# Row-sum guard, accumulator eviction, value products of 384 and 256 columns and the turning of the dense stage's tokens, changed together in a one-core transformer block

## The reference

```
q_rot, k_rot = (rotate(q), rotate(k))
scores = scale * np.matmul(q_rot, k_rot.transpose(0, 1, 3, 2))
attn = np.exp(scores - np.max(scores, axis=-1, keepdims=True))
attn = attn / (np.sum(attn, axis=-1, keepdims=True) + 1e-09)
x = np.matmul(attn, v)                         # then tokens x 512
...
h = np.maximum(x[mask] @ w1[e], 0.0)           # x 8 experts, one per token
y[mask] = gate_w[mask, None] * (h @ w2[e])
...
h = y @ w_in                                   # 512 -> 2048
return (h - np.tanh(h)) @ w_out                # 2048 -> 512
```

## Time and profile before

| | us |
|---|---|
| median of 3 runs | 1150.19 |
| lowest and highest run | 1147.87, 1151.51 |
| the profiled execution | 1149.18 |
| its span, first to last instruction | 1147.4 |
| attention, 0 to 377 | 377 |
| routing, 377 to 450 | 73 |
| experts, 450 to 704 | 254 |
| dense stage, 704 to the end | 443 |

### The profile page before, as it was taken

One profiled execution on the slowest core, in us unless ns is written; L12 is line 12 of the kernel. 1 busy time (PEld: TensorE's weight loads), 2 busy tenths in 40 slices (PEclk: granted clock), 3 DMA queues, 4 the chain that ended last, 5 costly groups with the idle time before them and its releaser, 6 DMA issues. The chain is left out here.

```text
span 1147.4 us, 18602 instructions
## 1 busy us (share of the span) xinstructions
PE 994.0 (87%) x5428; PEld 863.2 (75%) x5429; DVE 622.2 (54%) x1210; ACT 579.8 (51%) x1257; POOL 416.0 (36%) x246
## 2 busy tenths in 40 slices
PE   1988988888899108999999994999999999999996
PEld 1777877778788107888888873887988989889895
DVE  4677777777776433111111112776666666666664
ACT  2666666666665523222222223665556665555553
POOL 3988778768720164706975505000000000000000
PEclk9999999999999558999999997999999999999999
DMA  8776676666532165412542106121000000000001
GB/s 233 197 212 169 182 185 164 185 181 165 146 93 90 25 240 211 156 46 91 161 162 98 56 27 186 55 65 47 1 1 27 0 27 0 0 27 0 28 1 28
DMA packets 63077, 113.82 MB, mean 99 GB/s; under 512 B 20032, under 2 KB 24640, under 8 KB 61120
## 3 DMA queue, kind: packets, MB, share of 16 engines
q1 hardware_dynamic: 52352, 92.62, 27.8%
q10 hardware_dynamic: 7808, 11.31, 3.0%
q0 software_dynamic: 2880, 9.44, 2.4%
HBM read 60.58 MB, written 24.41 MB: 74 GB/s over the span
## 5 line engine op out<-in xcount | busy, mean ns | idle before, releaser
L1413 PE MATMUL hd_ps<-y_hi,w_hi 128*128 128x384 f32 x384 | 131.7, 343 | 4.9 <-DVE g_sb L1579 4.6
L601 DVE TENSOR_REDUCE neg_max<-ps 128x1 f32<-128x576 f32 x144 | 108.2, 751 | 40.3 <-PE ps L371 37.7
L1413 PE MATMUL hd_ps<-y_lo,w_hi 128*128 128x384 f32 x384 | 130.0, 339 | 0.0
L1413 PE MATMUL hd_ps<-y_hi,w_lo 128*128 128x384 f32 x384 | 129.8, 338 | 0.0
L1481 ACT ACTIVATE mag<-hd_ps 128x384 f32<-128x384 f32 x96 | 47.2, 492 | 159.8 <-PE hd_ps L1413 156.9
L1431 PE MATMUL o_ps<-w_hi,g_hi 128*128 128x512 f32 x288 | 114.9, 399 | 6.4 <-DVE g_lo L1588 5.7
L617 DVE TENSOR_TENSOR pt_lo<-ps,pt_hi 128x512 fp32r<-128x512 f32 x144 | 98.5, 685 | 39.9 <-ACT pt_hi L534 39.2
L514 ACT ACTIVATE probs<-ps,neg_max 128x576 f32<-128x576 f32 x128 | 95.4, 745 | 46.6 <-DVE neg_max L601 46.3
L1588 DVE TENSOR_TENSOR g_lo<-g_sb,g_hi 128x384 fp32r<-128x384 f32 x96 | 53.5, 557 | 116.8 <-ACT g_hi L1496 116.8
L534 ACT ACTIVATE pt_hi<-ps 128x512 fp32r<-128x512 f32 x144 | 86.8, 603 | 54.3 <-PE ps L418 54.2
L1431 PE MATMUL o_ps<-w_hi,g_lo 128*128 128x512 f32 x288 | 114.1, 396 | 0.0
(11 more groups left out here) (210 smaller groups left out, 2507.2 us busy)
## 6 DMA issues: line engine op xcount, KB each, us to landing
w_stage<-in_w SPq DMA_DIRECT2D x32, 512.0 KB, 3.8
raw_qk<-in_qk SPq DMA_DIRECT2D x14, 1152.0 KB, 6.1
k_hh<-qk_hi SPq DMA_DIRECT2D x64, 144.0 KB, 2.8
k_ll<-qk_lo SPq DMA_DIRECT2D x64, 144.0 KB, 2.9
sorted_rows<-zeros SPq DMA_DIRECT2D x28, 256.0 KB, 6.1
x_row<-sorted_rows ACTq DMA_DIRECT2D x20, 256.0 KB, 2.6
y_rows<-y_row ACTq DMA_DIRECT2D x20, 256.0 KB, 2.1
q_st<-qk_hi SPq DMA_DIRECT2D x32, 144.0 KB, 3.0
```

What stands on the lines that cost most here:

```text
L601: nc.vector.tensor_reduce(neg_max[r][:, i:i + 1], score[(r + i) % 2], AX.X, ALU.max, negate=True).then_inc(max_done, 1)
L1413: op = nc.tensor.matmul(hd_ps[f % 2][:, 0:G], w[:, c, cols], y[:, c, :], start=c == 0 and h == 0, stop=c == DC - 1 and h == 2)
```

## The change

Five edits:

1. The guard of the row sums. A tile `tiny` holds 1e-9, and `invert` adds it by a tensor_tensor instead of adding a constant by a tensor_scalar.
2. The layout of the turned probabilities and of the accumulator. `pt_hi` is one tile with 768 columns for each block: 128 tail columns of head A, 512 main columns, 128 tail columns of head B. The two buffers `pt_tail` and the `pt_corner` are gone; the tails lie at the ends (`ends`). The accumulator lies over two banks: 384 columns in one (A's tails and half of the main ones) and 384 in the next (the other half and B's tails). A value product is then four products: 384 and 256 columns with `hi` (256 and 384 for head B), and 256 and 256 with `lo`. MA, whose tail takes another weight, has five: 128, 256, 256, 256, 256.
3. The order of X and A0. A0 is turned in step 0 and X in step 1. As the tails have one buffer now, the rounding of X waits for B3 of the pair before.
4. The eviction. ACT evicts in step 6 (head A) and in step 1 of the next body (head B), behind the rounding of that step and ahead of its exponential.
5. The dense stage. `turn_y` is cut in two halves: chunks 0 and 1 in slice 13, ahead of `down(13)`, and chunks 2 and 3 in slice 14. ACT and DVE split the first half at the end of slice 13. `evac_o` comes behind `split_g`. `split_w(0)` comes ahead of `split_y(0)`.

```
             def turn(p, r, name, first=False):
-                before = {"A0": "", "X": "B3", "A1": "X", "A2": "A0", "C": "A1", "A3": "A2", "M": "C", "B0": "A3",
+                before = {"A0": "B3", "X": "", "A1": "A0", "A2": "X", "C": "A1", "A3": "A2", "M": "C", "B0": "A3",
                           "B1": "M", "B2": "B0", "B3": "B1"}[name]
-                if name == "X":
+                if name == "A0":
 
                     pe.wait_ge(exp_done, p * TILES + MIX + 1)
                     if not first:
 
                         pe.wait_ge(lo_done, p * UNITS)
-                elif name == "A0":
+                elif name == "X":
                     if not first:
 
...
-                pe.wait_ge(lo_done, p * UNITS + UNIT["M" if name[0] == "M" else name] + 1)
+                pe.wait_ge(lo_done, p * UNITS + UNIT["M" if name[0] == "M" else "X" if name == "A0" else name] + 1)
                 u = int("B" in name)
-                if name[0] == "M":
-                    buf, v_main, v_tail, tail = FULL, MIX + u, (TILES + 1, MIX + 1)[u], pt_corner[:, u, :, :]
-                else:
-                    buf = int(name[1])
-                    v_main = v_tail = buf + u * (MIX + 2)
-                    tail = pt_tail[r][:, buf, u, :, :]
+                k = FULL if name[0] == "M" else int(name[1])
+                main = v_split[r][:, MIX + u if name[0] == "M" else k + u * (MIX + 2), :]
                 begin, end = name in ("A0", "B0"), name[0] == "M"
-                nc.tensor.matmul(acc, v_split[r][:, v_main, :], pt_hi[buf][:], start=begin, stop=False)
-                nc.tensor.matmul(acc_tail, v_split[r][:, v_tail, :], tail.rearrange("p h s -> p (h s)"),
-                                 start=begin, stop=end)
-                nc.tensor.matmul(acc, v_split[r][:, v_main, :], pt_lo[buf][:], start=False,
-                                 stop=end).then_inc(pv_done, 1)
+                for a, z in ((P * u, P + MAIN // 2), (P + MAIN // 2, MAIN + P + P * u)):
+                    if name == "MA" and a == 0:
+                        nc.tensor.matmul(acc_tail[0], v_split[r][:, TILES + 1, :], pt_hi[:, k, 0:P], start=False,
+                                         stop=False)
+                        a = P
+                    nc.tensor.matmul(ps[:, CUT - MAIN // 2 - P + a:CUT - MAIN // 2 - P + z], main, pt_hi[:, k, a:z],
+                                     start=begin, stop=False)
+                for a, z in ((0, MAIN // 2), (MAIN // 2, MAIN)):
+                    last = nc.tensor.matmul(acc[:, a:z], main, pt_lo[:, k, a:z], start=False, stop=end)
+                last.then_inc(pv_done, 1)
...
-                elif not first and name != "X":
-
-                    act.wait_ge(pv_done, (p - 1) * VALUES + VALUE["MB" if name in "MC" else "B" + name[1]] + 1)
+                elif not first:
+                    last = {"X": "B3", "M": "MB", "C": "MB"}[name] if name in "XMC" else "B" + name[1]
+
+                    act.wait_ge(pv_done, (p - 1) * VALUES + VALUE[last] + 1)
...
             def body(p, r, first=False, second=False, last=False):
                 for i in range(TILES):
-                    if i == 2 and not first:
+                    round_hi(p, r, STEPS[i][0], first)
+                    if i == 1 and not first:
                         evac(p - 1, 1, second)
-                    if i == 7:
+                    if i == 6:
                         evac(p, 0, first)
-                    round_hi(p, r, STEPS[i][0], first)
                     if not last:
                         exp(p + 1, 1 - r, i)
                     for name in STEPS[i][1:]:
...
-                nc.vector.tensor_scalar(guarded[:], row_sum[r][:], 1e-9, None, ALU.add).then_inc(norm_step, 1)
+                nc.vector.tensor_tensor(guarded[:], row_sum[r][:], tiny[:], ALU.add).then_inc(norm_step, 1)
...
+            nc.vector.memset(tiny[:], 1e-9)
             nc.vector.memset(zeros[:], 0.0).then_inc(zero_set, 1)
+            dve.wait_ge(zero_set, 1)
...
                     elif not last:
                         if f + 2 == KF:
-                            turn_y(g + 1, False)
+                            turn_y(g + 1, False, (2, 3))
                         up(g + 1, f + 2 - KF, False)
+                    if f + 3 == KF and not last:
+                        turn_y(g + 1, False, (0, 1))
                     down(g, f, first)
...
@@ -1514,11 +1523,13 @@
                             split_w(f + 1)
                     elif not last:
                         read_h(g + 1, 0, False)
+                    if f == KF - 2 and not last:
+                        split_y(g + 1, (2, 3))
+                    split_g(g, f, first)
                     if f == 0 and not first:
                         evac_o(g - 1)
-                    split_g(g, f, first)
-                    if f == KF - 2 and not last:
-                        split_y(g + 1)
+                    if f == KF - 3 and not last:
+                        split_y(g + 1, (0, 1))
                     if f in (4, 7, 10) and not last:
                         gate_y(g + 1, (f - 4) // 3, second=first)
...
                 gate_y(0, i, True)
+            split_w(0)
             split_y(0)
             read_h(0, 0, True)
-            split_w(0)
             group(0, first=True)
...
```

More of the change, by code:

```diff
@@ L1388, in _, with turn_y @@
         def _(pe):
-            def turn_y(g, first):
-                pe.wait_ge(gated, g * GT + GT)
-                for c in range(DC):
+            def turn_y(g, first, chunks=range(DC)):
+                if 0 in chunks:
+                    pe.wait_ge(gated, g * GT + GT)
+                for c in chunks:
                     if not (first and c < 2):
```

46 lines of the change are left out of this document (24 added, 22 removed).

## The result

The changed kernel takes 1142.16 us (median of 6 runs, 1140.05 to 1143.42), the kernel before on the same chip 1150.78: a ratio of 0.9925, interval 0.9904 to 0.9946, 8.6 us less. Forecast were 1110, with a range to 1142, and as the first rival 1140. The kernel got faster by a fifth of the forecast gain (8.6 of 40 us), and the time lies just outside the range.

A forecast was written before the change was run, and what follows sets the result against it. Time was to come back where PE waits, most before MA behind the POOL-held guard. Guard 23.5, eviction 5, products 5 and dense stage 6.5 sum to 40 us: 1149.18 to 1109, median 1110; range 1098 to 1142.

The forecast's parts named there:

- first rival: Attention: the guard still waits for POOL, swallowing most of the eviction's and products' gains; 1140 us, chance 0.32.
- The guard: `invert` in attention: the new tensor_tensor no longer waits for POOL's instruction, saving 23.5 us; ends 0 and 23.5.
- phase: Attention: arriving 0.54 us earlier, the guard slips in ahead of L321 or into its gap and costs 0.16 us.
- main case: Whole kernel: the guard runs freely and all terms sum to 40 us, giving 1110 us; chance 0.50.
- The rule and rows 5: DVE beside POOL: two-SBUF-input instructions contend, the second blocking; routing's gather, started after DVE's L986, took 1.82 instead of 0.96 us.
- The eviction of head B: Attention, step 1: PE's 0.74 us wait before A0 goes, 0.4 returns before A1; 0.34 for 15 pairs, 5 us.
- Of head A: Attention, copies moved from step 7 to step 6: no slack before B3's turning, so counted at 0.
- The value products: Attention: a set falls from 0.68 to 0.62 us; 8.6 us over 144 sets, of which 5 were taken.
- rival 2: Value products: a set's fourth weight load shows, 24 us slower; chance 0.05, and 0.05 milder with a free guard.
- Dense stage: `evac_o` 4.5 us, the halves of `turn_y` 0, `split_w(0)` 2; together 6.5 us, ends −4 and 14.
- rival 3: Attention: an unseen wait, ACT before A1 or late stacks of q and k, cuts gains; 1120 to 1130, chance 0.08.

The follow-up runs named there:

- e3: The changed kernel with the tensor_scalar guard of the kernel before: 1141.65 us, ratio 0.9926.
- e2: The kernel before with only its guard left out (1e-9 not added): 1124.95 us, ratio 0.9782.
- e10: The kernel before with its guard left out and the eviction of head B moved to step 1: 1120.61 us, ratio 0.9733.
- e6: The changed kernel with the guard left out and the eviction of head A back in step 7: 1115.16 us, ratio 0.9647.
- e5: The changed kernel with `invert` ahead of the maximum of step 5 on DVE instead of behind it: 1124.07 us, ratio 0.9717.
- e4: The changed kernel with the eviction of head A back in step 7, head B's left in step 1: 1139.06 us, ratio 0.9899.
- e9: The changed kernel with a tensor_scalar guard whose result is written with a gap, and head A's eviction back in step 7: 1108.97 us, ratio 0.9636.
- e1: The changed kernel with the guard left out (1e-9 not added): 1110.36 us, ratio 0.9653.
- e7: The changed kernel with the guard as a tensor_scalar whose result is written with a gap: 1115.51 us, ratio 0.9649.
- e12: The changed kernel with `evac_o` ahead of `split_g` again: 1148.42 us, ratio 0.9982.
- e11: The changed kernel with all four chunks turned in slice 14 and `split_w(0)` behind `split_y(0)` again: 1145.19 us, ratio 0.9939.

## Why the prediction was wrong, step by step

- **The guard: the failed step.** I took 23.5 us "for a reason of phase that holds either way: the guard arrives 0.54 us into L321, and the changes ahead of it in the pair bring it forward by about 0.3 (first value products) + 0.3 (eviction)". The form of the instruction changed nothing (e3), so all hung on the phase. From POOL's restart behind MB to the guard it was 198.36 − 189.38 = 8.98 us before and is 220.74 − 212.15 = 8.59 after: 0.39 earlier (0.47 in every other pair), where 0.54 were needed and 0.6 counted. The term that was too large is that of the products: e2, e10 and e6 give 0.04 us to the new layout and order where I counted 0.3, and 0.41 to the eviction. So the guard comes 0.04 to 0.14 us too late and is held for nearly the whole of L322. In the two first pairs it did arrive late in an instruction and paid 0.48 and 0.79 us. The way out by the phase is real and nearly free: e3 has a guard of 0.16 us that starts 0.04 ahead of L322, and e5, brought forward further than needed, pays 0.5. I had built the main case on a margin of 0.06 us, against the only row on the form of the instruction.
- **The rule and rows 5 were right.** As the Trainium skill ("SBUF — State Buffer", § Who interferes with whom) has it, an instruction with two SBUF inputs is held by POOL's running instruction (2.60 us here), in the order that rows 5 had not shown. I gave this 0.32. With a margin of 0.06 us for the phase it should have been the forecast.
- **Rival 1 was right in kind and 5.6 us too kind to attention.** It let 3.5 us of the gain stay there, and everything ahead of the dense stage became 2.1 us longer; that its 1140 lies near 1142 is in part luck, since the dense stage gave 2.1 more than the 6.5 counted. All that was gained ahead of the guard went into a longer stall (2.13 to 2.56 us), and two costs came on top. The eviction in step 6 waits for MA, which the guard makes late, and puts 0.34 us more between the guard's end and MB in the pairs at full clock (e4). And behind 2.2 us of idle time PE ran at half its clock in every second pair, which costs that pair about 0.55 us; none of the kernels with a free guard shows this in the steady pairs.
- **The eviction of head B:** counted at 0.34 us a pair, measured at 0.40 (e2 to e10). About right in size, though in the changed kernel the stall swallowed it; and no wait before A1 of the 0.3 to 0.4 us that I counted shows in e10. **Of head A:** counted at 0, it costs 0.19 free (e6) and with the stall 0.34 in the pairs at full clock, 0.25 in the mean (e4). The step "I count 0" looked at what B0's wait could win and not at the exponential that stands behind the copies in step 6.
- **The value products:** a set is 0.05 us shorter, as argued; 0.20 us a pair reach the end (e10 to e6), 3 us where I took 5. No fourth weight load shows in a set of 0.63 us: rival 2 falls. The Trainium skill's estimate of a load, 107 ns ("TensorE: Matmul & The Clock Gate", § LDWEIGHTS (loading the stationary operand)), fits this better than the drawn 0.19 us.
- **Dense stage:** 6.5 expected, 8.6 measured: `evac_o` 5.7 (4.5), `split_w(0)` 2.1 (2), the turning 0.6 (0). For the first I took the wait, 0.86 us, for the whole loss, and a group gave 1.13. The stated ends of the three terms add up to −5 and 14, not −4 and 14, and the 1098 was worked out with 8 for this stage and not with its 14.
- **POOL, rival 3:** at 19.2 us a pair PE waited nowhere over 0.2 us in e9 and for no stack of q and k. With the guard free the whole sum comes out: e1 takes 1110.36 us, and 1110 was forecast. That is partly luck. Its terms measured 25.9 (guard), 6 (head B), −3 (head A), 3 (products) and 8.6 us (dense stage), against 23.5, 5, 0, 5 and 6.5, and their errors cancel.

## What to carry to other kernels

When a short DVE instruction ends together with a POOL instruction, pair after pair, suspect that it is held by it. In these runs its form decided then, not its size: look for a form beside the same POOL work that is not held (here the reciprocal behind it), and move the work into that form or to another engine. While such a hold pins the period, every gain ahead of it only makes the hold longer, and here the longer idle stretch came with lost clock too; so remove the hold first and measure the other edits behind it. A forecast that rests on a phase needs the distance from the event that restarts the other engine, and the share of each edit in it, to better than a tenth of a microsecond.

## What the runs showed of the hardware that was not expected

- The hold ends with each single POOL instruction, although the next follows within 0.1 us: 0.47 to 0.56 us in e5 to the end of L338. POOL itself loses nothing: L322 starts 2.73 us after L338 there (187.92 − 185.19), 2.75 in the changed kernel (198.75 − 196.00).
- A gap in the result's layout (three rows of three, pitch four) takes a tensor_scalar of 9 elements from 2.5 us to 0.15 beside the same POOL instruction (e3, e7).
- With an idle stretch of 2.1 to 2.25 us before MA, PE's granted clock fell to half for about 3 us in five to seven of eleven pairs between 80 and 320 us (changed kernel six, e3, e4 and e12 five, e11 seven). With 1.7 us (kernel before) it fell in one place, and with none of these stretches (e1, e2, e5 to e10) nowhere there. The drop follows now the stretches of 2.16 us (changed kernel) and now those of 2.24 (e3), so their length alone does not say which pair is hit.
